# Where the zero rows of each expert lie, and what the weight splits wait for

## The reference

```python
for t in range(S):                                   # attention
    cur = einsum('bhd,bhe->bhde', u[None] * k_t, v_t)
    y[:, :, t] = einsum('bhd,bhde->bhe', r_t, state + cur)
    state = w * state + einsum('bhd,bhe->bhde', k_t, v_t)
x = y as (3072, 384)
logits = x @ w_gate                                  # (3072, 8)
e = argmax(logits);  gate = softmax(logits)[e]
x = gate * (relu(x @ w1[e]) @ w2[e])                 # w1: 384 x 1024, w2: 1024 x 384
h = x @ w_in;  g = max(0.01 * h, h)                  # 384 x 2048
out = g @ w_out                                      # 2048 x 384
```

## Time and profile before

| | us |
|---|---|
| median of 3 runs | 893.01 (892.8 to 894.0) |
| profiled execution | 895.52 |
| its span, first to last instruction | 893.8 |
| mean granted clock of TensorE in it | 0.965 |
| PE busy | 821.3 (92%) |
| POOL busy | 360.3 (40%) |
| DVE busy | 378.2 (42%) |
| ACT busy | 227.4 (25%) |
| stores of zeros by ACT | 8, each 625.6 KB |

### The profile page before, as it was taken

One profiled execution on the slowest core, in us unless ns is written; L12 is line 12 of the kernel. 1 busy time (PEld: TensorE's weight loads), 2 busy tenths in 40 slices (PEclk: granted clock), 3 DMA queues, 4 the chain that ended last, 5 costly groups with the idle time before them and its releaser, 6 DMA issues.

```text
span 893.8 us, 13386 instructions
## 1 busy us (share of the span) xinstructions
PE 821.3 (92%) x4856; PEld 772.7 (86%) x4856; DVE 378.2 (42%) x706; ACT 227.4 (25%) x422; POOL 360.3 (40%) x376
## 2 busy tenths in 40 slices
PE   3899999992849999999997999999999999999996
PEld 3899998992749999998996998998998998998995
DVE  5767877773112322333126443343343343343322
ACT  1223334331111111121111223223223223223222
POOL 7685466454444787768769701001001001001001
PEclk9999999995788999999998999999999999999998
DMA  8546445502774554565364200000000000000000
GB/s 170 125 96 138 84 103 113 115 21 76 217 240 83 135 123 119 134 128 132 113 127 129 75 1 35 1 1 36 1 1 36 0 0 35 0 0 35 1 1 35
DMA packets 109952, 67.36 MB, mean 75 GB/s; under 512 B 85914, under 2 KB 103770, under 8 KB 109914
## 3 DMA queue, kind: packets, MB, share of 16 engines
q1 hardware_dynamic: 93005, 46.48, 22.4%
q10 hardware_dynamic: 13837, 10.92, 5.3%
q0 software_dynamic: 3072, 9.45, 2.8%
HBM read 51.62 MB, written 15.23 MB: 75 GB/s over the span
## 4 chain that ended last, share of the span: by engine, by line
PE 45%; POOL 18%; issue 8%; DMA 3%; POOLq 0%; SPq 0%; ACT 0%; DVE 0%
PE bank L1057 22%; PE bank L1036 22%; POOL w_lo L136 12%; POOL w_hi L132 5%; DMA stage<-in_moe_w 3%; POOL tick L122 1%; POOL out_rows L931 0%; DVE h_lo L1215 0%; POOLq L129 0%; POOLq L135 0%; SPq L883 0%; ACT hc L1137 0%; ACT h_hi L1141 0%; ACT rows L1150 0%; POOLq L936 0%
## 5 line engine op out<-in xcount | busy, mean ns | idle before, releaser
L931 POOL DMA_INDIRECT out_rows<-rows,ids_i x24 | 23.3, 972 | 357.2 <-ACT rows L1150 351.7
L1215 DVE TENSOR_TENSOR h_lo<-gf,h_hi 128x512 fp32r<-128x512 f32 x96 | 69.2, 721 | 225.4 <-ACT h_hi L1141 223.6
L136 POOL TENSOR_TENSOR w_lo<-stage,w_hi 128x768 fp32r<-128x768 f32 (+1 forms) x70 | 146.6, 2095 | 5.8
L1057 PE MATMUL bank<-w_hi,h_hi 128*128 128x384 f32 x384 | 129.8, 338 | 0.5 <-DVE h_lo L1215 0.5
L1057 PE MATMUL bank<-w_lo,h_hi 128*128 128x384 f32 x384 | 128.9, 336 | 0.0
L1057 PE MATMUL bank<-w_hi,h_lo 128*128 128x384 f32 x384 | 128.6, 335 | 0.0
L1137 ACT ACTIVATE hc<-bank 128x512 f32<-128x512 f32 x96 | 57.4, 598 | 274.2 <-PE bank L1036 274.2
L1036 PE MATMUL bank<-x_hi,w_hi 128*128 128x512 f32 x288 | 112.9, 392 | 5.8 <-POOLq L142 5.8
L1036 PE MATMUL bank<-x_lo,w_hi 128*128 128x512 f32 x288 | 113.9, 395 | 0.0
L1036 PE MATMUL bank<-x_hi,w_lo 128*128 128x512 f32 x288 | 113.5, 394 | 0.0
L1179 DVE SCALAR_TENSOR_TENSOR h_lo<-bank,h_hi 128x416 fp32r<-128x416 f32 x64 | 37.8, 592 | 150.9 <-ACT h_hi L1111 150.9
(11 more groups left out here) (143 smaller groups left out, 1390.7 us busy)
## 6 DMA issues: line engine op xcount, KB each, us to landing
stage<-in_moe_w SPq DMA_DIRECT2D x24, 512.0 KB, 6.3
stage<-in_moe_w SPq DMA_DIRECT2D x32, 384.0 KB, 3.2
rows<-x_rows ACTq DMA_DIRECT2D x9, 625.6 KB
x_rows<-pad_row ACTq DMA_DIRECT2D x8, 625.6 KB
rn<-in_r SPq DMA_DIRECT2D x48, 96.0 KB, 2.4
kn<-in_k SPq DMA_DIRECT2D x48, 96.0 KB, 2.6
vp<-in_v SPq DMA_DIRECT2D x48, 96.0 KB, 2.6
stage<-in_moe_w_in SPq DMA_DIRECT2D x6, 512.0 KB, 4.3
```

The costliest lines, as they stand in the source:

```text
L136: i = eng.tensor_tensor(w_lo[:, buf, off:off + cols], stage[:, h, 0:cols], w_hi[:, buf, off:off + cols].bitcast(F32), ALU.subtract)
L931: pool.indirect_dma_start(out, bass.IndirectOffsetOnAxis(ap=idx.bitcast(U32), axis=0), rows[:, t, 0:D], None).then_inc(stored, 16)
L1057: i = pe.matmul(ps_o[t][:, 0:D], x[:, f % NB, t * P:(t + 1) * P], ww[:, 1, o:o + D], start=f == 0 and x is h_hi and ww is w_hi, stop=f == ...
L1215: dve.tensor_tensor(h_lo[:, f % NB, :], gf[:, f % 2, :], h_hi[:, f % NB, :].bitcast(F32), ALU.subtract).then_inc(gl_ok, 1)
```

## The change

The rows of an expert now lie behind a block of zero rows, not in front of one. A region begins with 416 zero rows (`zero_rows`), stored by SP in the first stage, one expert after each of the first eight `reload`s. Tokens are placed from row U of the region on (`region_no` starts at U). A group is counted from the expert's last row back, so that its surplus rows are the zero rows or rows of the same expert that another group has too. `z_t` and `id_rows` are filled from the end to the front, and the dense stage takes its groups from the end. ACT's `pad`, its waits and the table `end_i` go; the table at the end of the routing has other arithmetic (`cum_s`, `cmp_s`, `slot_c`).

POOL's wait ahead of a weight set is divided: the three pieces of the first layer wait for the `hidden` steps of the group that used the buffer (`h_mm`), the four of the second layer for its `output` steps. The pieces of `w_in` are ordered by halves of its 2048 columns, and so are their places in the buffer. The first three wait for `h_mm`, the others for `l2_mm`, `parts_ready` is incremented after three and after six, and PE waits for the first half before `layer1` step 0 and for the second before step 8.

```diff
     def w_in_pieces():
-        return [(c * FD + h * PIECE, PIECE, moe2_w_in[c * P:(c + 1) * P, h * PIECE:(h + 1) * PIECE].unsqueeze(1))
-                for c in range(DC) for h in range(FD // PIECE)]
+        return [((h * DC + c) * PIECE, PIECE, moe2_w_in[c * P:(c + 1) * P, h * PIECE:(h + 1) * PIECE].unsqueeze(1))
+                for h in range(FD // PIECE) for c in range(DC)]
...
+                def zero_rows(e):
+                    dst = x_rows[e * RR:e * RR + U, :].rearrange("(t p) d -> p t d", p=TR)
+                    sp.dma_start(dst, pad_row[0:TR, :].unsqueeze(1).broadcast_to([TR, U // TR, XW])).then_inc(filled, 16)
 
                 sp.wait_ge(consts, 11)
-                sp.dma_start(x_rows[0:U, :].rearrange("(t p) d -> p t d", p=TR),
-                             pad_row[0:TR, :].unsqueeze(1).broadcast_to([TR, U // TR, XW])).then_inc(filled, 16)
                 for c in range(2):
                     for q in range(HP):
                         reload(c, q)
                         n = c * HP + q
+                        if n < E:
+                            zero_rows(n)
                         if 2 <= n < 6:
                             issue_piece(sp, n, n % 2, pc[n])
...
-                pool.iota(region_no[:, :], [[RR, E]], base=0, channel_multiplier=0).then_inc(consts, 1)
+                pool.iota(region_no[:, :], [[RR, E]], base=U, channel_multiplier=0).then_inc(consts, 1)
...
-                pool.wait_ge(filled, 16)
...
+                dve.tensor_tensor(cum_s[:, :], x, tl[:, :], ALU.subtract)
...
+                dve.tensor_tensor(cmp_s[:, :, :], slot_n[:, :].unsqueeze(2).broadcast_to([P, LOOKS, E]),
+                                  cum_s[:, :].unsqueeze(1).broadcast_to([P, LOOKS, E]), ALU.is_ge)
...
+                dve.tensor_tensor(cmp_s[:, :, :], cmp_s[:, :, :], cnt[:, :].unsqueeze(1).broadcast_to([P, LOOKS, E]),
+                                  ALU.mult)
...
-                dve.tensor_copy(end_i[:, :], run[:, 0, :])
...
+                dve.tensor_reduce(slot_c[:, :], cmp_s[:, :, :], AX.X, ALU.add)
                 link(dve.tensor_tensor(slot_t[:, :], slot_n[:, :], slot_t[:, :], ALU.subtract))
-                link(dve.tensor_scalar(slot_t[:, :], slot_t[:, :], float(U), None, ALU.mult))
-                dve.scalar_tensor_tensor(slot_r[:, :], slot_e[:, :], float(RR), slot_t[:, :], ALU.mult, ALU.add)
-                link(dve.tensor_tensor(slot_o[:, :], slot_o[:, :], slot_t[:, :], ALU.add))
-                dve.tensor_scalar(group_off[:, :], slot_o[:, :], float(N), None, ALU.min)
+                dve.tensor_scalar(slot_r[:, :], slot_e[:, :], float(RR), None, ALU.mult)
+                link(dve.scalar_tensor_tensor(slot_o[:, :], slot_t[:, :], float(U), slot_o[:, :], ALU.mult, ALU.add))
+                dve.tensor_scalar(slot_t[:, :], slot_o[:, :], -1.0, float(N), ALU.mult, ALU.add)
+                link(dve.tensor_tensor(slot_c[:, :], slot_c[:, :], slot_o[:, :], ALU.subtract))
+                dve.tensor_scalar(group_off[:, :], slot_t[:, :], 0.0, None, ALU.max)
+                link(dve.tensor_tensor(slot_r[:, :], slot_r[:, :], slot_c[:, :], ALU.add))
                 link(dve.tensor_tensor(group_row[:, :], slot_r[:, :], valid[:, :], ALU.mult))
...
                 def weights(n, b):
-                    if not isinstance(n, int):
-
-                        pool.wait_ge(l2_mm, n * FC - FC)
-                        carry_wait(pool, 2)
                     for i, piece in enumerate(expert_pieces(0)):
+                        if not isinstance(n, int) and i in (0, DC):
+
+                            pool.wait_ge(l2_mm if i else h_mm, n * FC - FC)
+                            carry_wait(pool, 2)
                         split_piece(pool, n * NPE + i, (b * NPE + i) % 2, b, piece, i in ENDS)
...
-                pool.wait_ge(l2_mm, last * FC)
-                carry_wait(pool, 2)
                 for n, piece in enumerate(w_in_pieces()):
-                    split_piece(pool, base + n, n % 2, 0, piece, n == NPI - 1)
+                    if n in (0, DC):
+
+                        pool.wait_ge(l2_mm if n else h_mm, last * FC)
+                        carry_wait(pool, 2)
+                    split_piece(pool, base + n, n % 2, 0, piece, n in (DC - 1, NPI - 1))
...
+                    if isinstance(g, int) and g == 0 and f in (0, FFC // 2):
+
+                        pe.wait_ge(parts_ready, pairs * 4 + (2 if f else 1))
...
-                pe.wait_ge(parts_ready, pairs * 4 + 1)
...
                 def group(n, b):
-                    first = isinstance(n, int) and n == 0
...
-                    if not first:
-                        load_x(n + 1)
-                        move_ids(n)
+                    load_x(n + 1)
+                    move_ids(n)
                     for f in range(FC):
                         act.wait_ge(h_mm, n * FC + (f + 1))
                         act.activation(h_hi[:, f % NB, 0:U], ps_h[f % 2][:, 0:U], ACT.Relu).then_inc(h_hi_ok, 1)
-                        if first and f < E // 2:
-                            pad(2 * f)
-                            pad(2 * f + 1)
-                    if first:
-                        act.wait_ge(padded, 16 * E)
-                        load_x(1)
-                        move_ids(0)
...
                     for d in range(DC):
-                        z = z_t[:, d, g * (G * P):(g + 1) * (G * P)] if isinstance(g, int) else \
-                            z_t[:, d, bass.ds(g * (G * P), G * P)]
+                        at = (NG - 1 - g) * (G * P) + U
+                        z = z_t[:, d, at:at + G * P] if isinstance(g, int) else z_t[:, d, bass.ds(at, G * P)]
```

More of the change, by code:

```diff
@@ L195, in build_program @@
             cum = sb("cum", [P, 2, E], stack=st1)
+            cum_s = sb("cum_s", [P, E], stack=st1)
+            cmp_s = sb("cmp_s", [P, LOOKS, E], stack=st1)
+            slot_c = sb("slot_c", [P, LOOKS], stack=st1)
             total_i = sb("total_i", [P, 1], I32, stack=st1)
@@ L929, in scatter @@
                             pool.wait_ge(o_dve, g * 2 + t - 1)
-                        idx = ids_i[:, g * G + t:g * G + t + 1]
+                        m = (NG - 1 - g) * G + t
+                        idx = ids_i[:, m:m + 1]
                         pool.indirect_dma_start(out, bass.IndirectOffsetOnAxis(ap=idx.bitcast(U32), axis=0),
```

12 lines of the change are left out of this document (3 added, 9 removed).

## The result

The changed kernel took 879.54 us (median of 4, 876.69 to 882.38) against 893.5 (4 runs, 892.8 to 894.85) for the kernel before: a ratio of 0.9842, 95% interval 0.9807 to 0.9877. Forecast were 873.5 and the range 866 to 881. The profiled execution took 882.38 (span 880.6), 13.1 less than that of before, where the sum had said 19.5. On two other chips the ratio was 0.9789 (0.9732 to 0.9846) and 0.9855 (0.9823 to 0.9888).

A forecast was written before the change was run, and what follows sets the result against it. PE bounds the kernel nearly everywhere. The third dense slice comes 21.0 us sooner, less 1.2 of slow clock and 0.3 in the first stage: 19.5, so 893.0 becomes 873.5; range 866 to 881, its own 870 to 877.

The forecast's parts named there:

- Part 1: Zero rows stored early: 10.8 us of wait, 2.2 for `h_lo` and 2.2 of slow clock go, sum 15.2.
- +0.3: First stage: eight zero stores added on SP's queue cost 0.3 us, between bounds of 0 and 24.
- Part 3: Weight-set waits by layer and half: POOL starts group 2's set 19.5 us sooner; PE's 5.82 us dense wait goes.
- the 4.1 us: Experts, group 6: PE's 2.33 us wait for second-layer weights and slow matmuls behind it, 4.1 us, would go.
- rival B: Experts: POOL's chain falls behind again; one late piece costs 4.1 us, two 8.2: 877.6 and 881.7; chance 0.17.
- a sign that the prediction had named for being wrong: PE waits at L1001 in groups 5 to 7 were listed among what would show the forecast wrong.
- The dense start: PE begins its third dense slice at 464.5, 21.0 us sooner, after DVE's split taking 10.6 us.
- The 5.3 us: Dense start: it would come 5.3 us sooner than forecast without GpSimd and VectorE sharing a port pair.
- rival A: Dense start: DVE slips through while POOL waits for a DMA; 26.8 us gained, 866.5 in all; chance 0.14.
- The rest of the dense stage: Behind the dense start, PE at full clock keeps its length: no change forecast.
- C: First stage: zero stores push each unit's loads onto the path, 3.0 us eight times: 897.5, slower; chance 0.03.
- D: First load behind group 0 still late, 10.8 + 2.2 stay, POOL's early start idle: about 889; chance 0.04.

The follow-up runs named there:

- e3: Changed kernel with the old waits of the weight sets, PE waiting for all six pieces of `w_in`: 869.12 us, ratio 0.9805 to the kernel before.
- e5: Changed kernel with token numbers moved by SP after its last weight piece, not by ACT in each group: 871.43 us, ratio 0.9804.
- e7: Changed kernel with POOL holding from the fifth piece of `w_in` until DVE has split the first dense tokens: 873.32 us, ratio 0.9811.
- e9: Changed kernel with the table `end_i` declared again at its old place and never used: 870.38 us, ratio 0.9814.
- e4: Kernel before with only the new waits by layer and half, padding kept: 887.24 us, ratio 1.0008.
- e11: Changed kernel with id moves last on SP, zero stores away from scatters, POOL holding ahead of `w_out`, and the unused table: 864.46 us, ratio 0.9759.
- e10: Changed kernel with id moves last on SP, zero stores away from scatters, and POOL holding ahead of `w_out`: 865.29 us, ratio 0.9766.

## Why the prediction was right, and where it wasn't

**Part 1, the padding: right in mechanism, a little small in size.** Forecast: 10.8 us of wait, 2.2 of waits for `h_lo`, 2.2 of slow clock, 15.2 together. From group 0's first `x_hi` copy to group 1's it is 26.93 instead of 42.08, so 15.15 by itself; the next interval gives another 1.5 (28.91 instead of 30.44), 16.7 in all. The load is issued 24 us before PE wants its rows (235.20 to 259.49, the start of the transposes). The load and the id move ahead of group 0's first relu cost nothing that shows.

**The zero stores: the transfer right, the bill short of one wait.** The DMA share between 50 and 60 us was forecast at 0.81 and is 0.76:

```profile
50.00:60.00 10.00, 9.61 (x89) 9.45 (x88) 7.10 (x11) 3.44 (x7) 9.12 (x8) 1.00 0.76 177
```

I had listed what is queued behind a store, and left out who shares the DMA engines with it without being queued: POOL's scatter, whose landing POOL and, through DVE, PE wait for. That is the step that failed. The wait in chunk 2 was not there before and is 3.0 to 4.25 us in all seven profiles with this first stage. By itself it costs nothing; in the recorded profile PE stood 1.92 us for it and then ran at half clock for some 10 us, and that made +0.3 into +5.0. In those seven profiles (the changed kernel three times, `e3`, `e5`, `e7`, `e9`) the first load comes at 226.1, 223.8, 220.4, 221.05, 221.0, 221.2 and 219.9 against 221.1 before. The middle one is 221.05, so +0.3 was right for the usual execution, and the recorded one is the worst. What makes the 223.8 is the half clock between 44 and 52 us, before the first scatter.

**Part 3, the 4.1 us: the cause wrong, the size right in two of three profiles.** I gave the end of POOL's late pieces to the new waits. Undoing them changes nothing that shows (`e3`), and alone they gain nothing that the times show (`e4`). POOL's 13.61 us of waiting were made by the padding, and part 1 takes them away with it. The 4.1 us were counted once, so the sum did not suffer, but they were credited to the wrong edit. In the recorded profile two late pieces cost 5.6 us, which is rival B; the two other profiles of the changed kernel have none in these groups. Rival B's price (877.6 to 881.7) is where the recorded median fell, and in the profiled execution it came together with the late first load; the other three executions of that median have no profile. PE's waits in groups 5 and 6 are a sign that the prediction had named for being wrong.

**The dense start: right in number, in part by luck.** Forecast was the third slice at 464.5 with DVE's split as the last thing; it began at 469.32, and without the 5.0 us of the first stage that is 464.3. Errors cancel in it. The late pieces took 5.6 us that were not forecast. Against that the split took 7.8 us and not 10.6, part 1 gave 1.5 more, and five groups came 27.98 and not 28.22 us apart, 1.2 together. The 5.3 us that the prediction names for a start without contention leave out the 1.7 us of slow matmuls that its rival A counts. The Trainium skill's rule on the shared ports ("SBUF — State Buffer", "Who interferes with whom") holds, by `e7`: 3.3 us alone.

**The rest of the dense stage: wrong by 2.7 us.** I wrote that it keeps its length. The spacing of the first layer's matmuls depends on where the buffers lie, and the change took out a table of 32 bytes per partition (`e9`). With the table back the stage is 407.60 in `e11` but 409.74 in `e9`, so that this is all of the 2.7 us is not shown.

**Rivals.** A (DVE slips through) happened only where POOL was made to wait. C (stores in series) is refuted: 24 us were its price, and the median of seven profiles shows none. D is refuted by the 26.93 us between the first two groups.

**The forecast against the three ratios.** 0.9842, 0.9789 and 0.9855 of 893.0 are 878.9, 874.2 and 880.1; the forecast of 873.5 lies below all three. The recorded median of 879.54 is inside the range of 866 to 881, but outside the 870 to 877 that were given as the forecast's own. It is inside because the range had been drawn out for rival B. The base may be part of it: 19.5 us were the sum against one profile of before, and by `e4` some of its 8.1 us of waits for POOL may not be there in other executions. Its mean granted clock, 0.965, is also lower than in all but two of the 31 executions beside the experiments (those took 893.84 and 895.18 us). That the base is the cause was not shown.

## What to carry to other kernels

When a transfer is added, list not only what is queued behind it but every wait for a landing that shares the DMA engines with it, and the slack of each. Follow the wait to TensorE: what it costs there can be a stretch at half clock, longer than the wait. When a stage is late, look at the granted clock in it before a wait is blamed. When an engine's wait is about to be credited to an edit, ask first whether the other edit that makes its releaser earlier removes it anyway. And a hold that frees a port pays only where the engine that holds has slack: in `e7` POOL's 6.7 us came back as a wait of 4.0 and a half clock behind it, in `e10`, with the id moves gone and the hold ahead of `w_out`, its 7.0 us cost nothing.

## What the runs showed of the hardware that was not expected

- An unused table of 32 bytes per partition ahead of the buffers moves matmul spacing by about 1%, and not the same way in both stages: 27.98 us without it and 28.22 with it for a group, 231.8 ns without it and 229.9 or 230.1 with it in the dense stage's first layer.
- Moves of 416 elements of 4 bytes between two places in DRAM (1.6 KB, 7.3 us from issue to landing in `e5`) hold up 384 and 512 KB weight pieces on another queue: POOL waits 27.8 to 35.9 us for pieces in three profiles of the changed kernel and 23.1 to 23.9 in the three in which the moves come last.
- A wait for a scatter to land is free up to 3.4 us here. Behind the two longer ones (4.25 and 4.73) TensorE, having stood 1.92 and 1.36 us, ran at a granted clock of 0.50 for 8 and 11 us, and the first load came 5.0 and 8.1 us later.
- The same six VectorE instructions beside a splitting GpSimd took 6.5, 7.8 and 9.2 us in three profiles of one kernel, and 3.3 with GpSimd still.
